# Sums over k tiles that hold one batch each: 65 columns in place of 130 in the attention stage of a fused kernel

## What is computed

```python
# q, k, v: (4 batches, 8 heads, 576 tokens, 64); omega: (128 features, 64)
def phi(x):
    proj = einsum('bhsd,md->bhsm', x, omega)
    h = proj - sum(x * x, axis=-1, keepdims=True) / 2
    h = h - max(h, axis=-1, keepdims=True)
    return exp(h) / sqrt(m)
q_p, k_p = phi(q * scale), phi(k * scale)
kv = einsum('bhsm,bhsd->bhmd', k_p, v)     # sums over the tokens of one batch and head
z = sum(k_p, axis=2)
num = einsum('bhsm,bhmd->bhsd', q_p, kv)
den = einsum('bhsm,bhm->bhs', q_p, z)[..., None] + 1e-06
attn = num / den
x = moe(attn); out = moe2(x)               # the dense layer, then the experts
```

## Time and profile before

| | |
|---|---|
| median of 3 runs (lowest to highest) | 822.8 us (822.49 to 823.07) |
| profiled execution, its time | 821.22 us |
| its span | 819.4 us |
| PE busy over the span | 776.6 us (95%) |
| DVE, ACT, POOL busy | 356.1, 309.6, 331.0 us |
| 288 matmuls of the sums (L254) | 37.9 us busy |
| attention, to the first matmul of the dense layer | 155.95 us |

### The profile page before, as it was taken

How to read it: one execution, slowest core, us unless ns; L and a number is a source line. 1 busy time by engine, 2 the same in 40 slices (tenths; PEclk the granted TensorE clock), 3 DMA queues, 4 the chain that set the end, 5 groups by cost and what they waited for, 6 DMA issues and landing times.

```text
span 819.4 us, 15712 instructions
## 1 busy us (share of the span) xinstructions
PE 776.6 (95%) x5502; PEld 711.2 (87%) x5503; DVE 356.1 (43%) x904; ACT 309.6 (38%) x718; POOL 331.0 (40%) x282
## 2 busy tenths in 40 slices
PE   5899989999999999999999999996999999999993
PEld 5777777889899989989989998995999999999993
DVE  5767777611224424433443446653762322332231
ACT  3777777633232242232233223262224424325220
POOL 5677777035312222222222223265026726528411
PEclk9999999999999999999999999998999999999997
DMA  7876674011050020020002001321061632521111
GB/s 263 300 259 228 229 254 170 2 52 52 0 181 0 1 77 0 0 77 0 0 0 77 0 0 40 123 84 48 21 236 58 190 119 89 186 58 29 37 49 31
DMA packets 25156, 74.17 MB, mean 91 GB/s; under 512 B 3088, under 2 KB 3216, under 8 KB 24992
## 3 DMA queue, kind: packets, MB, share of 16 engines
q1 hardware_dynamic: 21856, 63.68, 22.1%
q0 software_dynamic: 3264, 10.03, 4.1%
HBM read 61.11 MB, written 12.58 MB: 90 GB/s over the span
## 4 chain that ended last, share of the span: by engine, by line
PE 73%; issue 10%; POOL 9%; ACT 4%; DVE 3%; DMA 1%; ACTq 0%; SPq 0%; DVEq 0%; POOLq 0%
PE pj L675 21%; PE nm L862 14%; PE pj L1268 8%; PE kv L862 7%; PE kv L1284 6%; PE nm L1284 6%; PE nm L1268 5%; POOL sqt L192 2%; POOL sqt L188 2%; POOL gl L832 2%; PE pj L1297 1%; PE tr L1255 1%; ACT feat L388 1%; POOL W L1090 1%; DMA qk<-in_qk_n 1%
## 5 line engine op out<-in xcount | busy, mean ns | idle before, releaser
L832 POOL TENSOR_TENSOR gl<-g,gh 128x384 fp32r<-128x384 f32 x96 | 100.8, 1053 | 297.9 <-ACT gh L693 297.9
L688 DVE TENSOR_TENSOR g<-pj,sg 128x384 f32<-128x384 f32 x96 | 53.5, 558 | 223.6 <-ACT sg L683 223.4
L683 ACT ACTIVATE sg<-pj 128x384 f32<-128x384 f32 x96 | 47.2, 492 | 253.6 <-PE pj L675 253.6
L675 PE MATMUL pj<-xh,win_h 128*128 128x384 f32 x384 | 129.5, 337 | 1.2 <-DVE xl L710 1.2
L675 PE MATMUL pj<-xh,win_l 128*128 128x384 f32 x384 | 129.4, 337 | 0.0
L675 PE MATMUL pj<-xl,win_h 128*128 128x384 f32 x384 | 128.9, 336 | 0.0
L675 PEld LDWEIGHTS pj<-xh,win_h 128*128 128x128 f32 x384 | 72.2, 188 | 5.2 <-DVE xl L710 1.5
L675 PEld LDWEIGHTS pj<-xl,win_h 128*128 128x128 f32 x384 | 72.1, 188 | 3.6
L675 PEld LDWEIGHTS pj<-xh,win_l 128*128 128x128 f32 x384 | 72.0, 188 | 0.0
L1268 PE MATMUL pj<-xTh,W 128*128 128x288 f32 x320 | 70.4, 299 | 0.0
L798 DVE SCALAR_TENSOR_TENSOR raw<-tr,xT 128x512 f32<-128x512 f32 x90 | 58.6, 689 | 8.8 <-DVE g L688 8.1
(11 more groups left out here) (243 smaller groups left out, 1724.9 us busy)
## 6 DMA issues: line engine op xcount, KB each, us to landing
wraw<-in_moe_w SPq DMA_DIRECT2D x7, 2048.0 KB, 10.8
ve<-in_v_z SPq DMA_DIRECT2D x16, 585.0 KB, 3.8
qk<-in_qk_n SPq DMA_DIRECT2D x16, 576.0 KB, 4.8
qkT<-in_qk_t SPq DMA_DIRECT2D x16, 576.0 KB, 5.1
y_rows<-ys SPq DMA_DIRECT2D x18, 256.0 KB, 2.3
stage<-in_moe_w_in SPq DMA_DIRECT2D x8, 512.0 KB, 6.1
y_early<-ys SPq DMA_DIRECT2D x12, 256.0 KB, 2.7
stage<-in_moe_w_out SPq DMA_DIRECT2D x4, 512.0 KB, 5.6
```

Source lines behind the costliest of these rows:

```text
L675: mm = eng.matmul(ph[f % 3][:, 0:BT], w[f // F1A][:, c, f % F1A, :], x[:, c, :], start=(c == 0 and w is win_h and x is xh), stop=(c == DC ...
L683: eng.activation(sg[f % 2][:, :], ph[f % 3][:, 0:BT], ACT.Sigmoid, scale=1.702).then_inc(a_sg, 1)
L688: eng.tensor_tensor(g32[f % 2][:, :], ph[f % 3][:, 0:BT], sg[f % 2][:, :], ALU.mult).then_inc(v_g, 1)
L832: eng.tensor_tensor(gl[f % 3][:, :], g32[f % 2][:, :], gh[f % 3][:, :].bitcast(F32), ALU.subtract).then_inc(g_gl, 1)
```

## The change

Each unit's k and v tokens are laid out anew. Tile 0 keeps 64 tokens of either batch (the last 64 of 576), the four tiles 1 to 4 hold the first 512 tokens of batch 0, the four tiles 5 to 8 those of batch 1. q's tiles stay as they were. The sums' first matmul still has 130 columns. The eight others have 65, and go to the half of the bank that belongs to their batch. `ve` holds no zeros for these eight: a partition's row in it falls from 9 x 130 to 130 + 8 x 65 = 650 values. The layout is made on the host, as it was before.

```diff
+KT = (RJ - 1) // 2
+VZ = 2 * KT * HW + VW
...
-    ve = [at(f"ve{a}", [P, RJ, VW], 49152 + 4704 * a) for a in range(2)]
+    ve = [at(f"ve{a}", [P, VZ], 49152 + 2624 * a) for a in range(2)]
...
-            eng.dma_start(ve[a][:, :, :].rearrange("p j c -> p (j c)"),
-                          v_z[bass.ds(i, 1), :, :].rearrange("i p r -> (i p) r")).then_inc(ld_v[a], 16)
+            eng.dma_start(ve[a][:, :], v_z[bass.ds(i, 1), :, :].rearrange("i p r -> (i p) r")).then_inc(ld_v[a], 16)
...
-            for j in range(RJ):
-                mm = eng.matmul(kv[:, 0:VW], feat[a][:, j, :], ve[a][:, j, :],
-                                start=(j == 0), stop=(j == RJ - 1))
+            eng.matmul(kv[:, 0:VW], feat[a][:, 0, :], ve[a][:, 0:VW], start=True, stop=False)
+            for t in range(2 * KT):
+                b = t // KT
+                mm = eng.matmul(kv[:, b * HW:(b + 1) * HW], feat[a][:, 1 + t, :], ve[a][:, VW + t * HW:VW + (t + 1) * HW],
+                                start=False, stop=(t == 2 * KT - 1))
             mm.then_inc(p_kv, 1)
```

More of the change, by code:

```diff
@@ L1728, in units, with tiles_k @@
         return x.reshape(2, 2, HEADS, HD, RJ, HD).transpose(0, 2, 1, 3, 4, 5).reshape(UNITS, P, RJ, HD)
-    qk = np.concatenate([units(k), units(q)], axis=2)
-    qk_t = qk.reshape(UNITS, P, PG, 2, GT, HD).transpose(0, 3, 5, 2, 4, 1)
-    v_z = np.zeros((UNITS, P, RJ, VW), np.float32)
+    def tiles_k(x):
+        y = x.reshape(2, 2, HEADS, SEQ, HD).transpose(0, 2, 1, 3, 4).reshape(UNITS, 2, SEQ, HD)
+        whole = y[:, :, :KT * P].reshape(UNITS, 2 * KT, P, HD).transpose(0, 2, 1, 3)
+        return whole, y[:, :, KT * P:].reshape(UNITS, P, HD)
+    whole, mixed = tiles_k(k)
+    qk = np.concatenate([mixed[:, :, None], whole, units(q)], axis=2)
+    qk_t = qk.reshape(UNITS, P, PG, 2, GT, HD).transpose(0, 3, 5, 2, 4, 1)
+    whole, mixed = tiles_k(v)
+    v_z = np.zeros((UNITS, P, VZ), np.float32)
+    by_tile = v_z[:, :, VW:].reshape(UNITS, P, 2 * KT, HW)
+    by_tile[..., :HD] = whole
+    by_tile[..., HD] = 1.0
+    v_z[:, :, VW:] = by_tile.reshape(UNITS, P, 2 * KT * HW)
     om_2 = np.concatenate([omega.T, omega.T])
     for h in range(2):
-        rows = slice(HD * h, HD * h + HD)
-        v_z[:, rows, :, HW * h:HW * h + HD] = units(v)[:, rows]
-        v_z[:, rows, :, HW * h + HD] = 1.0
+        rows, at = slice(HD * h, HD * h + HD), HW * h
+        v_z[:, rows, at:at + HD] = mixed[:, rows]
+        v_z[:, rows, at + HD] = 1.0
     return {"qk_t": qk_t.reshape(UNITS, P, T2 * P), "qk_n": qk.reshape(UNITS, P, 2 * RJ * HD),
-            "v_z": v_z.reshape(UNITS, P, RJ * VW), "om_2": om_2}
+            "v_z": v_z, "om_2": om_2}
 def kernel(**inputs):
```

## The result

The changed kernel takes 824.28 us (median of 20 runs, 821.28 to 825.63), the kernel before 821.88 us (20 runs, 820.0 to 823.87). The ratio is 1.0027, with an interval of 1.0017 to 1.0036: a loss of 0.27% where a gain of as much was forecast, and outside the range.

The account below looks back on a forecast made before the run. A circle through ACT, POOL, DVE and one PE `turn_x` bounds the loop; PE's sums count at start and end. Gains 0.9 + 0 + 1.3 = 2.2 us take 822.8 to 820.6 us; range 819.5 to 823.0.

Parts of the forecast that it names:

- Pitch: In each set of sums, matmuls would follow at 0.057 us in place of 0.112, saving 0.88 us a set.
- rival 1: In the sums, loads of 128 weights set the pitch, not columns, so it stays: 822.8 us; chance 0.08.
- Start: In step 0, shorter sums bring POOL's first `low` about 0.9 us earlier, range 0.4 to 1.1.
- Rival 3: At the start, the clock rises some 2 us later over shorter matmuls, losing the gain: 821.5 to 821.8 us; chance 0.09.
- Loop: In steps 2 to 12, no gain of its own; the two-step round stays 18.4 us.
- Rival 2: In the loop, odd steps gain 0.78 us in six rounds, 4.7 us more: 815.8 us; chance 0.08.
- Rival 5: In the loop, PE idles about 1.8 us, its clock falls, adding 19 us: about 840 us; chance 0.05.
- End: In steps 13 and 14, PE's earlier sums bring the dense layer 1.32 us earlier, lower end 0.9.
- Behind the attention: The dense layer and the experts move by the attention's gain of 2.2 us, unchanged.

Follow-up runs that it names:

- half weights: Changed kernel, seven of every eight 65-column sums using only the first 64 features as weights, giving wrong sums: 906.39 us, ratio 1.103.
- before, 17 spares: Kernel before plus spare matmuls with unused results, 12 before the first projection and 5 ahead of the third: 821.71 us, 0.9999.
- padded transfers: Changed kernel with 65-column matmuls, each load of ve padded with unread values to the old 585 KB: 824.30 us, 1.0036.
- changed, 17 spares: Changed kernel plus spare matmuls with unused results, 12 before the first projection and 5 ahead of the third: 823.46 us, 1.0019.
- 26 spares: Spare matmuls at the start (12, then 10, and 4 in step 0) added to the kernel before: 820.88 us, 0.9983; to the changed one: 820.58 us, 0.9982.

## Why the prediction was wrong

**Pitch: 0.057 us forecast, 0.112 measured. This is the step that failed, and rival 1, with a chance of 0.08, was right about it** (not about the time, which it put at no change). The step took its price from the outputs, whose pairs stream 65 columns and load 2 x 64 weights in 0.057 us, and treated one load of 128 weights as two of 64. It is not: loads of 64 weights go at 0.058 us each with 65 columns (half weights, all in one column half), loads of 128 at 0.112 with 65 columns as with 130. The outputs, of the same shape as the half weights but in both column halves in turn, go at 0.028, their records starting in twos 0.007 us apart: the two halves take their loads side by side, each at 0.057. A load of 128 weights covers both halves and was not faster than 0.112 in any run. The argument that 0.057 is half of 0.112 should have been read as half the weights just as well as half the columns. What the earlier trace rows held was one shape in which both were halved.

The Trainium skill has the rule, in "TensorE: Matmul & The Clock Gate", section "LDWEIGHTS (loading the stationary operand)": a load takes the number of weight columns over 1.2 in ns, whatever the rows. By it 128 columns take 107 ns and 64 take 53. At the upper level the pitches agree within 6 ns (0.112 and 0.058 us). At the lower level they do not: 128 weights follow each other at 0.213 us there with 65 columns and at 0.217 with 130, and 64 weights at 0.11, twice the rule, which names no level. The prediction weighed the same page's 81 ns for a pair of load and matmul; no trace here shows that figure for 128 weights of fp32.

**Start: 0.9 us of gain forecast, 2.0 to 2.5 us of loss against the trace of before in four traces of five.** With the pitch unchanged there was nothing to gain. But the step also fixed the rise of the clock at 18.35 us. In the traces in which PE runs the start of step 0 at the lower level or only just behind it, with 128 weights throughout, the first `low` and the clock's last rise ahead of it came at (the rises from the trace's list of clock changes):

| sums of step 0 | kernel | first `low` | last rise | ratio |
|---|---|---|---|---|
| 130 columns | before | 26.04 | 18.4 | 1 |
| 130 | all 130 in the new layout | 24.42 | 15.2 | 1.0002 |
| 130 | step 0 alone | 27.02 | 20.2 | 0.9998 |
| 130 | before, 17 spares | 26.09 | 18.7 | 0.9999 |
| 65 | changed | 24.64 | 15.4 | 1.0027 |
| 65 | changed, run again | 28.27 | 23.5 | 1.0021 |
| 65 | padded transfers | 28.49 | 24.2 | 1.0036 |
| 65 | step 0 alone | 28.00 | 22.8 | 1.0038 |
| 65 | changed, 17 spares | 28.35 | 23.4 | 1.0019 |

The rise varies in both groups. With 65 columns four traces of five show it at 22.8 or later, with 130 none later than 20.2. The five ratios of the lower group lie between 1.0019 and 1.0038, and none of their intervals reaches 1; those of the upper one lie at 1 to within 0.0002, with intervals of about 0.0013 to either side. Rival 3 had this mechanism and put it at 2 us, with the gain at the end left over; it sized the cost of the delay at less than half and had no gain to lose.

The same page of the Trainium skill says, in its section "Seeing it yourself", that the recorded events of the clock have been seen to be unreliable, and advises a cross-check. The cross-check paid here, though for another reason. With the column at 1.00, the step 0 of the kernel narrowed there alone has 13 matmuls in 2 us, as the changed kernel run again has with the column at 0.50. But the recorded events themselves agree with every record that could be compared; what misleads is the column ahead of the first event.

**Loop: nothing, right.** The round is 18.38 us in the changed kernel, and also with half the weights, where a set is 0.46 us shorter. Rival 2 fell by that. Rival 5 fell too, up to the gap that this run made: project 2 at 72.59 follows 1.11 us of idling in place of the 0.16 in the earlier trace rows, and still takes 0.94 us, its length at the upper level. A gap of 1.8 us in the loop was never made. At the start, 2.04 and 0.92 us of idling with a projection of 0.94 us between them were enough for the clock to fall (the changed kernel run again), so that a gap of that size in the loop is no safe bet.

**End: 1.3 us forecast, 0.13 measured.** From the first `low` to the dense layer it is 129.86 to 129.92 us in the five traces whose later sums have 130 columns (before, new layout, both kernels of before with spares, step 0 alone at 65), and 129.71 to 129.80 in the seven that have 65. The means, 129.90 and 129.77, differ by 0.13 us. The rule of the prediction, twice the saving of a set as long as that is under 0.54 us, gives 0.12 for the 0.06 us that a set really saved. With half the weights it gives 2 x 0.46 = 0.92, and 0.94 was measured. The rule held; its term was mis-sized by the pitch.

Two slips of addition change nothing: by the prediction's own numbers the projection of the start comes at 17.82 us (not 17.85) and rival 2 at 815.9 us (not 815.8).

**Behind the attention: "moves unchanged" was too simple.** The trace of the changed kernel enters the gap at the gathers earlier, and the clock falls in it as in the earlier trace rows. PE then starts earlier but works longer at the lower level. The fifth multiplication of line 873 (877 in the changed kernel) stands last in each of these two timelines, before and then changed:

```profile
567.64 0.53 PE L862 MATMUL kv<-wb_h,gh 128*128 128x512 f32 x1
...
569.39 0.39 PE L873 MATMUL nm<-wb_l,gh 128*128 128x512 f32 x1
```
```profile
562.74 0.74 PE L1259 MATMUL tr<-ident,xb 96*128 96x96 f32 x3 [6.22 <-DMA xb<-y_early,gcol]
...
568.02 0.56 PE L877 MATMUL nm<-wb_h,gl 128*128 128x512 f32 x1
...
568.65 0.40 PE L877 MATMUL nm<-wb_l,gh 128*128 128x512 f32 x1
```

The transposes lead by 564.49 - 562.74 = 1.75 us, that multiplication by only 569.39 - 568.65 = 0.74. The rise comes at 567.9 and 568.4, nearly the same time, while PE had begun 1.75 us sooner. At the last transposes of the kernel the changed one leads by 0.80 us still (807.19 against 807.99), and this goes too. The very last ones:

```profile
809.58 0.64 PE L1297 MATMUL pj<-ident,yTs 128*96 128x128 f32 x4 [0.94 <-DVE ob L1473]
```
```profile
809.15 1.09 PE L1301 MATMUL pj<-ident,yTs 128*96 128x128 f32 x4 [0.94 <-DVE ob L1477]
```

0.64 us before and 1.09 in the changed kernel, whose clock had fallen at 807.3, and 1.02 in place of 0.64 for those before them. So the same two spans of 819.4 us hold different things, and a lead won at the start can be lost twice later. The stretch at the lower level behind the gap also has no fixed length: 561.1 to 567.9 us in the trace of before, 558.1 to 568.4 in that of the kernel before with 26 spares, whose span is 819.5 us although its attention is 2.07 us shorter. With that stretch filled the ratio is 0.9957 in place of 0.9982. This is more than the start's lead of some 2 us (0.9973 at best), since the kernel before pays for that stretch too.

**What stays open.** Why the clock rises later when the sixteen matmuls of step 0 stream half as many columns. The first of them starts between 15.5 and 16.1 us at either width, and they load as many weights at nearly the same pitch (0.213 and 0.217 us at the lower level); only the columns differ. No run tells which property of the work the chip goes by. The two traces with half the weights, whose 65 columns follow each other twice as fast, have their last rise at 17.2 and 23.9 us, one in the range of either group, and settle nothing. How often the rise is early or late is known from one trace per kernel (two of the changed one); the medians suggest only that it is late more often with 65 columns. The loss of the medians (2.4 us in 821.88) and the delay of the late traces (2.0 to 2.5 us) agree, but that the one is the other execution by execution was not shown.

## What to carry to other kernels

Before you count columns saved, look at what sets the pitch: halve weights and columns apart, and take the price of a narrower matmul only from a row with the same weights. Work that looks wasted, here zeros streamed in the first microseconds, can go with an earlier rise of TensorE's clock; keep it in the first step, or fill PE's idle time there with spare matmuls. Where a kernel's start lies under a clock that rises at varying times, compare medians and several traces, never two spans.

## What the runs showed of the hardware

- Loads of 128x128 weights in fp32 with a matmul of 65 or of 130 columns behind each follow each other at 0.112 us at the upper level (2.4 GHz) and at 0.213 and 0.217 us at the lower (1.2 GHz). With 64 weight columns and 65 streamed it is 0.058 us at the upper level and 0.11 at the lower. In no run did 64 weights meet 130 columns.
- After 2.10 us of idling at 9.5 to 11.6 us the clock, up since the first spares, fell at about 12 us (the kernel before with 17 spares); with the idle time cut to 0.98 us by more spares it stayed up, in the trace of the kernel before with 26:

```profile
11.87 0.94 PE L242 MATMUL pj<-om,qkT 64*128 64x128 f32 x12 [0.98 <-ACT feat L398]
```

- 26 spare matmuls at the start, which hold the projection ahead of the sums back by 0.08 us at most (1.95 us behind the one before it in place of 1.87), give 0.9982 to 0.9983; 22 more ahead of the gathered rows, in a gap of about 6 us, bring it to 0.9957.
- The column of the granted clock reads 1.00 ahead of the trace's first clock change, even where every record is as long as at the lower level (7 to 22 us in the kernel narrowed in step 0 alone). There the lengths of the records decide.
